# A kernel of attention, SoLU block and mixture of experts: sums and loads of attention moved, tiles turned by halves of their rows

## The reference

```python
# attention: q, k, v are (4, 8, 1152, 64); query pairs are averaged, so 576 queries a head
q_pool = q.reshape(B, H, S // 2, 2, D).mean(axis=3)
scores = scale * np.matmul(q_pool, k.transpose(0, 1, 3, 2))
attn = softmax(scores)                       # with + 1e-09 in the denominator
x = np.matmul(attn, v)                       # then (2304, 512): tokens x features
# SoLU block: w_in (512, 1024), w_out (1024, 512)
h = x @ w_in
solu = h * softmax(h)
x = (layer_norm(solu) * g_ln) @ w_out
# experts: 8 of them, w1 (512, 1024) and w2 (1024, 512) each, a token goes to the best one
out[mask] = gate_w[mask, None] * (np.maximum(x[mask] @ w1[e], 0.0) @ w2[e])
```

## Time and profile before

| | |
|---|---|
| median of 3 runs | 1072.29 us (1070.62 to 1072.95) |
| the profiled execution | 1071.67 us |
| its span, first to last instruction | 1069.6 us |
| mean granted TensorE clock | 0.986 of full |
| busy: TensorE, VectorE, ScalarE, GpSimd | 1012.2, 689.1, 605.1, 409.8 us |

### The profile page before, as it was taken

How to read it: one execution, slowest core, us unless ns; L and a number is a source line. 1 busy time by engine, 2 the same in 40 slices (tenths; PEclk the granted TensorE clock), 3 DMA queues, 4 the chain that set the end, 5 groups by cost and what they waited for, 6 DMA issues and landing times.

```text
span 1069.6 us, 23686 instructions
## 1 busy us (share of the span) xinstructions
PE 1012.2 (95%) x8139; PEld 713.1 (67%) x8139; DVE 689.1 (64%) x1461; ACT 605.1 (57%) x1356; POOL 409.8 (38%) x566
## 2 busy tenths in 40 slices
PE   8699999999999999989999999997999999999996
PEld 5355555555555555545888888876778888888884
DVE  5477777777777777865589999997855513233110
ACT  5477777777777777754654434444556524333231
POOL 3556666565556656673222221152021121111100
PEclk9799999999999999999999999998999999999999
DMA  3432333333332322314300000053665713311100
GB/s 105 110 79 73 83 88 78 88 87 82 84 86 71 81 78 62 108 24 157 91 21 21 30 21 21 21 187 99 245 238 190 269 50 120 119 41 32 40 21 2
DMA packets 97518, 93.66 MB, mean 88 GB/s; under 512 B 49966, under 2 KB 70446, under 8 KB 97264
## 3 DMA queue, kind: packets, MB, share of 16 engines
q1 hardware_dynamic: 93392, 80.79, 25.3%
q0 software_dynamic: 4000, 11.28, 3.2%
HBM read 74.73 MB, written 11.27 MB: 80 GB/s over the span
## 4 chain that ended last, share of the span: by engine, by line
PE 46%; DVE 3%; issue 2%; ACT 1%; POOL 1%; DMA 1%; DVEq 0%; ACTq 0%; POOLq 0%
PE h_ps L771 9%; PE h_ps L773 9%; PE h_ps L772 9%; PE o_ps L771 5%; PE o_ps L773 5%; PE o_ps L772 5%; PE t_ps L1252 2%; PE t_ps L1142 1%; PE h_ps L1219 1%; DVE junk L1348 1%; DMA w_raw_e<-in_moe_w 1%; PE h_ps L1268 1%; DVE w_split L1566 0%; POOL x_lo L1051 0%; ACT w_split L1747 0%
## 5 line engine op out<-in xcount | busy, mean ns | idle before, releaser
L719 ACT ACTIVATE probs<-s_ps,lows 128x576 f32<-128x576 f32 x272 | 199.2, 737 | 88.0 <-DVE lows L603 86.9
L392 POOL TENSOR_SCALAR probs<-probs,raises,recips 128x576 f32<-128x576 f32 x272 | 220.7, 829 | 71.5 <-DVE recips L625 71.5
L603 DVE TENSOR_REDUCE lows<-s_ps 128x1 f32<-128x576 f32 x288 | 204.9, 751 | 62.9 <-PE s_ps L515 55.4
L515 PE MATMUL s_ps<-kt,qt 64*128 64x288 f32 x1024 | 163.2, 435 | 11.1 <-ACT probs L719 9.7
L515 PEld LDWEIGHTS s_ps<-kt,qt 64*128 64x128 f32 x1024 | 88.2, 188 | 113.8 <-ACT probs L719 94.9
L554 PE MATMUL pv_ps<-pt,values 128*64 128x512 f32 x576 | 156.3, 622 | 0.3 <-DVE x_t L647 0.2
L1070 POOL DMA_INDIRECT out<-junk,target_rows x25 | 28.8, 1152 | 261.8 <-ACT junk L1785 261.5
L469 PE MATMUL t_ps<-ident,probs 64*128 64x64 f32 x2178 | 118.9, 226 | 7.4 <-ACT pt L714 5.4
L469 PEld LDWEIGHTS t_ps<-ident,probs 64*128 64x128 f32 x2178 | 104.5, 140 | 22.4 <-DVE pt L632 17.9
L632 DVE COPY pt<-t_ps 128x512 f32<-128x512 f32 x144 | 98.5, 684 | 7.2 <-PE t_ps L469 6.8
L1348 DVE SCALAR_TENSOR_TENSOR junk<-x_rows,emb 128x512 f32<-128x512 f32 x128 | 94.4, 791 | 0.1
(11 more groups left out here) (281 smaller groups left out, 2099.4 us busy)
## 6 DMA issues: line engine op xcount, KB each, us to landing
w_raw_e<-in_moe_w SPq DMA_DIRECT2D x60, 512.0 KB, 5.6
k_raw<-in_k SPq DMA_DIRECT2D x32, 256.0 KB, 2.6
q_raw<-in_q SPq DMA_DIRECT2D x32, 256.0 KB, 3.3
qt<-qx SPq DMA_DIRECT2D x60, 128.0 KB, 2.4
token_rows<-x_rows SPq DMA_DIRECT2D x18, 256.0 KB, 2.0
values<-in_v SPq DMA_DIRECT2D x32, 128.0 KB, 2.7
values<-in_v SPq DMA_DIRECT2D x64, 64.0 KB, 2.6
w_raw<-in_moe_w_in SPq DMA_DIRECT2D x4, 512.0 KB, 5.7
```

Of the source, the lines that this page charges most:

```text
L392: nc.gpsimd.tensor_scalar(where, where, raises[:, par, s, c:c + 1], recips[:, par, s:s + 1], ALU.mult, ALU.mult).then_inc(norm_done if c e ...
L515: last = nc.tensor.matmul(s_ps[c][:, u, 0:part], qt[par][rows(u), s, :], kt[par][rows(u), int(s > full), columns(c)], start=True, stop=True)
L603: nc.vector.tensor_reduce(lows[:, g % 2, s, c:c + 1], s_ps[c][:, :, 0:part], AX.XY, ALU.max, negate=True).then_inc(low_done[c], 1)
L719: nc.scalar.activation(two_halves(probs(g, s)[:])[:, :, columns(c)], s_ps[c][:, :, 0:part], ACT.Exp, bias=lows[:, g % 2, s, c:c + 1], scal ...
```

## The change

In attention the product and the sum of the totals move from GpSimd to VectorE, and the addition of 1e-9 goes into the sum. VectorE now waits for `raises_done` itself, and GpSimd for the reciprocals alone. In VectorE's slot 0 the totals of the last batch of the pair before are written ahead of the loop over batches; no batch has its merge or its totals in slot 0, so the order of what is executed stays. SyncE loads the queries and their tails of pair n first, then the keys of the first head, moves the queries, loads the tail of the keys, the values, and the keys of the second head.

In SoLU and in the experts a tile is turned in 16 transposes of 64 rows by 128 columns instead of 8 of 128 by 128, upper and lower row half in turn. Rows are tokens, so one bank of `t_ps` now holds tokens 0 to 63 of all eight feature blocks, and the other tokens 64 to 127. ScalarE and VectorE copy out by token halves, in strips of 64, into the same `y_hi` and `y_lo`. Both banks are signalled at once. So ScalarE's first copy waits for the whole product of the tile before, the turn for both subtractions of the tile before, and a product for both subtractions of its own tile.

```diff
@@ sync, attention loop
                 if n < pairs:
+                    sp.wait_ge(q_sums, sum_count(n - 1, Q))
+                    load_q(n, 0)
+                    load_q(n, 1)
+                    sp.wait_ge(q_sums, sum_count(n - 1, TAILS))
+                    load_q_tail(n)
                     sp.wait_ge(kq_done, kq_count(n - 1, KA))
                     load_a(n)
                 if at + 1 < pairs:
                     move_queries(at + 1)
+                if n < pairs:
+                    sp.wait_ge(kq_done, kq_count(n - 1, TAILS))
+                    load_k_tail(n)
                 if at < pairs:
                     if at >= 2:
                         sp.wait_ge(pv_done, key_tiles * (at - 1))
                     load_values(at)
                 if n < pairs:
-                    sp.wait_ge(q_sums, sum_count(n - 1, Q))
-                    load_q(n, 0)
-                    load_q(n, 1)
-                    sp.wait_ge(kq_done, kq_count(n - 1, TAILS))
-                    load_k_tail(n)
-                    sp.wait_ge(q_sums, sum_count(n - 1, TAILS))
-                    load_q_tail(n)
                     sp.wait_ge(kq_done, kq_count(n - 1, KB))
                     load_b(n)
@@ gpsimd, normalise
-                steps = 2 * (len(batches) * g + b)
-                pool.wait_ge(raises_done, len(batches) * g + b + 1)
-                pool.sem_inc(passed, 1)
-                nc.gpsimd.tensor_tensor(weighted[:, par, first:end, :], raises[:, par, first:end, :],
-                                        sums[:, par, first:end, :], ALU.mult).then_inc(total_steps, 1)
-                pool.wait_ge(total_steps, steps + 1)
-                pool.sem_inc(passed, 1)
-                nc.gpsimd.tensor_tensor(total[:, par, first:end], weighted[:, par, first:end, 0],
-                                        weighted[:, par, first:end, 1], ALU.add).then_inc(total_steps, 1)
                 pool.wait_ge(recips_done, len(batches) * g + b + 1)
@@ vector, invert_totals
-                dve.wait_ge(total_steps, 2 * (len(batches) * g + b) + 2)
-                nc.vector.tensor_scalar(total[:, par, first:end], total[:, par, first:end], 1e-9, None,
-                                        ALU.add).then_inc(guarded, 1)
-                dve.wait_ge(guarded, len(batches) * g + b + 1)
+                n = len(batches) * g + b + 1
+                dve.wait_ge(raises_done, n)
+                nc.vector.tensor_tensor(weighted[:, par, first:end, :], raises[:, par, first:end, :],
+                                        sums[:, par, first:end, :], ALU.mult).then_inc(weighted_done, 1)
+                dve.wait_ge(weighted_done, n)
+                nc.vector.scalar_tensor_tensor(out=total[:, par, first:end], in0=weighted[:, par, first:end, 0],
+                                               scalar=1e-9, in1=weighted[:, par, first:end, 1], op0=ALU.add,
+                                               op1=ALU.add).then_inc(total_done, 1)
+                dve.wait_ge(total_done, n)
                 nc.vector.reciprocal(recips[:, par, first:end], total[:, par, first:end]).then_inc(recips_done, 1)
@@ build_moe
+        def blocks_of(y, u):
+            return y[:].rearrange("p (b u n) -> p u b n", u=2, n=P // 2)[:, u, :, :]
+
+        def turned_of(u):
+            return t_ps[:, u, :].rearrange("p (b n) -> p b n", n=P // 2)
@@ tensor, down
-                pe.wait_ge(y_lo_done, 2 * m + half + 1)
+                pe.wait_ge(y_lo_done, 2 * m + 2)
@@ tensor, turn and turn_h
+            def turn_by_halves(source, done):
+
+                for f in range(ff_blocks):
+                    for u in range(2):
+                        rows = slice(u * P // 2, (u + 1) * P // 2)
+                        last = nc.tensor.transpose(t_ps[:, u, f * P // 2:(f + 1) * P // 2],
+                                                   source[rows, f * P:(f + 1) * P], ident[rows, rows])
+                last.then_inc(done, 2)
+
             def turn(m):
                 pe.wait_ge(y_ready, m + 1)
-                for half in range(2):
-                    if m >= 1:
-                        pe.wait_ge(y_lo_done, 2 * m - 1 + half)
-                    for i in range(ff_blocks // 2):
-                        f = half * ff_blocks // 2 + i
-                        done = nc.tensor.transpose(t_ps[:, half, i * P:(i + 1) * P],
-                                                   solu[:, m % 2, f * P:(f + 1) * P], ident[:])
-                    done.then_inc(turned, 1)
+                if m >= 1:
+                    pe.wait_ge(y_lo_done, 2 * m)
+                turn_by_halves(solu[:, m % 2, :], turned)
@@ scalar, high_y (low_y, high_h and low_h in the same way)
                 if m >= 1:
-                    act.wait_ge(down_done if half else down_half_done, m)
-                nc.scalar.activation(y_hi[:, half_of(half)], t_ps[:, half, :], ACT.Copy).then_inc(y_hi_done, 1)
+                    act.wait_ge(down_done, m)
+                nc.scalar.activation(blocks_of(y_hi, half), turned_of(half), ACT.Copy).then_inc(y_hi_done, 1)
```

More of the change, by code:

```diff
@@ L154, in build_attention @@
         raises_done = sem("raises_done")
-        total_steps = sem("total_steps")
-        guarded, recips_done = sem("guarded"), sem("recips_done")
+        weighted_done, total_done, recips_done = sem("weighted_done"), sem("total_done"), sem("recips_done")
         half_scaled = sem("half_scaled")
@@ L652, in _ @@
                         lowest(at, s, 1)
+                    if s == 0 and 1 <= at <= pairs:
+                        invert_totals(at - 1, len(batches) - 1)
+                    if at < pairs:
                         for b, (first, end) in enumerate(batches):
@@ L657, in _ @@
                                 invert_totals(at, b)
-                    if s == 0 and 1 <= at <= pairs:
-                        invert_totals(at - 1, len(batches) - 1)
                     if i is not None:
@@ L1245, in turn_h @@
             def turn_h(t):
-                for half in range(halves):
-                    pe.wait_ge(relu_done, halves * t + half + 1)
-                    if t >= 1:
-                        pe.wait_ge(h_lo_done, halves * (t - 1) + half + 1)
-                    for i in range(ff_blocks // 2):
-                        f = half * ff_blocks // 2 + i
-                        done = nc.tensor.transpose(t_ps[:, half, i * P:(i + 1) * P], h[:, f * P:(f + 1) * P], ident[:])
-                    done.then_inc(h_turned, 1)
+                pe.wait_ge(relu_done, halves * (t + 1))
+                if t >= 1:
+                    pe.wait_ge(h_lo_done, halves * t)
+                turn_by_halves(h, h_turned)
             def down_e(t, expert, slot):
@@ L1258, in down_e @@
                     pe.wait_ge(y_copied, t - 1)
+                pe.wait_ge(h_lo_done, halves * (t + 1))
                 for f in range(ff_blocks):
-                    if f % (ff_blocks // 2) == 0:
-                        pe.wait_ge(h_lo_done, halves * t + f // (ff_blocks // 2) + 1)
                     blk, cols = slice(f * P, (f + 1) * P), slice(f % 2 * d_model, (f % 2 + 1) * d_model)
@@ L1377, in low_y @@
                 dve.wait_ge(y_hi_done, 2 * m + half + 1)
-                nc.vector.tensor_tensor(y_lo[:, half_of(half)], t_ps[:, half, :], y_hi[:, half_of(half)].bitcast(F32),
+                nc.vector.tensor_tensor(blocks_of(y_lo, half), turned_of(half), blocks_of(y_hi, half).bitcast(F32),
                                         ALU.subtract).then_inc(y_lo_done, 1)
@@ L1614, in low_h @@
                     dve.wait_ge(h_hi_done, halves * t + n + 1)
-                    nc.vector.tensor_tensor(y_lo[:, half_of(n)], t_ps[:, n, :], y_hi[:, half_of(n)].bitcast(F32),
+                    nc.vector.tensor_tensor(blocks_of(y_lo, n), turned_of(n), blocks_of(y_hi, n).bitcast(F32),
                                             ALU.subtract).then_inc(h_lo_done, 1)
@@ L1777, in high_h @@
                         act.wait_ge(down_e_done, t)
-                    nc.scalar.activation(y_hi[:, half_of(n)], t_ps[:, n, :], ACT.Copy).then_inc(h_hi_done, 1)
+                    nc.scalar.activation(blocks_of(y_hi, n), turned_of(n), ACT.Copy).then_inc(h_hi_done, 1)
             def scale(t):
```

## The result

The changed kernel is slower: a median of 1081.62 us (1080.13 to 1083.39, four runs) beside 1072.45 us of the kernel before on the same chip, a ratio of 1.0089 with an interval of 1.0070 to 1.0109. The forecast was 1051. The profiled execution has a span of 1080.1 us against 1069.6, that is, 10.5 us more.

What follows compares the result with a forecast made beforehand. TensorE was taken to set the pace, losing time in attention to VectorE's waits for GpSimd's totals. The terms -10 - 8 - 3.5 + 0.5 = -21 took 1071.67 to 1051 us; 8-in-10 range 1042 to 1062.

Steps and rivals of the forecast that it cites:

- Start of attention, -10: At the start of attention, queries loaded earlier end the wait for q_sum: -10 us, bounds -8.5 and -11.
- Steady pairs, -8: In attention's steady head pairs, sums on VectorE shorten TensorE's 0.90 us stop: -8 us, bounds 0 and -13.
- last pair, -3.5: In attention's last pair, TensorE's 1.94 us stop and the slow work behind it go: -3.5 us, bounds 0 and -4.
- rival 3: In attention, VectorE's new operations stand behind GpSimd's scalings, so the steady 8 us don't come: 1059 us, chance 0.13.
- Part 3: SoLU and expert turns by row halves: gain 0.17 us a turn, bounds 0 and 0.36, 37 turns, -6.3 us.
- if half turns take over 0.87: Sign that the forecast is wrong: a SoLU or expert half turn, expected at 0.70 us, takes over 0.87.
- parts 3 and 4: SoLU and experts, turning by row halves and handing over whole tiles together: +0.5 us, bounds -6.5 and +7.
- Part 4, tail, +4.7: SoLU's tail: whole-tile hand-over delays the last products and the routing, +4.7 us.
- first SoLU tiles, +1.5: SoLU's first tiles: ScalarE's copy and square come behind the whole product, +1.5 us.
- last expert tile, +0.6: Last expert tile: the product waits for a second subtraction, 0.68 less an overlap of 0.08, +0.6 us.
- Rival 4: SoLU's whole-tile hand-over overruns its 5.6 us cover, so TensorE stops every tile: 1077 us, chance 0.05.

Runs made afterwards that it cites:

- the loads alone: The kernel before with only the changed order of SyncE's loads: 1066.22 us, ratio 0.9939.
- the sums alone: The kernel before with only attention's sums and reciprocals on VectorE, loads in the order of before: 1057.09 us, ratio 0.9850.
- the registers first: The changed kernel with TensorE reading a tile's two registers ahead of the expert turn: 1061.01 us, ratio 0.9900.
- both mends: The changed kernel with expert register reads ahead of the turn and SoLU's last two tiles turned and handed over as before: 1053.02 us, ratio 0.9828.

## Why the prediction was wrong, point by point

- **Start of attention, -10.** The score expected at about 34 came at 35.00, the one expected at 38.6 at 39.96, and 45.98 follows without a low clock. By the rest product the gain is 8.8 us, within the bounds (-8.5 to -11). The split between the parts was not forecast; the runs give 6.0 to the loads alone and 4.0 to the sums alone (63.09), and not quite their sum to both.
- **Steady pairs, -8, and last pair, -3.5.** Right in kind: the 0.90 us stop went, one to two new operations were blocked, and the stop of 0.33 became 0.45 to 0.56 where it occurs (0.68 once, at 449.35), with 0.5 forecast. Since it is absent in five pairs, the gain is 0.9 a pair rather than 0.63: 12.6 us over fourteen intervals, the last pair's first part among them, near the upper bound. From there to the first mark 1.25 us were gained, so the last pair gave less than 3.5 by itself. The sum of attention, -22.6 against -21.5, came out near partly by luck: the start gave 1.2 less than forecast, the steady pairs 4.6 more and the last pair 2.25 less.
- **The blocked operations (rival 3).** The rule of the Trainium skill (SBUF — State Buffer, section "SBUF: two separate sides"), that two such operations lock each other out for a whole instruction, agrees with the 0.62 to 0.77 us above, and with 0.16 where GpSimd stood idle. But it didn't decide: VectorE has room once its wait is gone, as the forecast chose.
- **Part 3, 0.17 a turn: failed.** In SoLU, where nothing else changes, the tile went from 12.07 to 12.04. The marks were unlike. The 0.87 of a full turn runs from its start to where the next product's pace is regular, with the slow step at its end in it; for the half turn I took 0.65 of attention, which has neither edge, and added 0.05. Counted from the last regular product before to the first one behind, less two steps of 0.233, a full turn is 608.72 - 607.38 - 0.466 = 0.87, a half turn 599.39 - 598.08 - 0.466 = 0.84.

Before:

```profile
607.38 0.39 PE L773 MATMUL o_ps<-w_hi,y_lo 128*128 128x512 f32 x1
607.61 1.04 PE L1142 MATMUL t_ps<-ident,solu 128*128 128x128 f32 x8
608.40 0.47 PE L771 MATMUL o_ps<-w_hi,y_hi 128*128 128x512 f32 x1
608.72 0.39 PE L772 MATMUL o_ps<-w_lo,y_hi 128*128 128x512 f32 x1
```

After:

```profile
598.08 0.40 PE L770 MATMUL o_ps<-w_hi,y_lo 128*128 128x512 f32 x1
598.41 0.71 PE L1143 MATMUL t_ps<-ident,solu 64*128 64x64 f32 x16
599.05 0.51 PE L768 MATMUL o_ps<-w_hi,y_hi 128*128 128x512 f32 x1
599.39 0.39 PE L769 MATMUL o_ps<-w_lo,y_hi 128*128 128x512 f32 x1
```

So the turn itself is 0.15 shorter (0.64 against 0.79), and the entry gives 0.10 of it back (0.33 against 0.23). The edge behind it is 0.34 against 0.32. 37 turns are worth 1 us and not 6.3; the measured value lies within the bounds (0 to 0.36), at their foot. The sign of being wrong, "if half turns take over 0.87", did not show: they take 0.84, and that is hardly less.

- **Not in the sum at all: the register reads.** I listed what `turn_h` and `up_e` compute, wait for and hand over, and left out the two reads between them, since the trace of before shows no time for them. That was the missing step: 23 stops of some 0.95, the 22 us of the experts. Part 3 made the turn shorter in time and doubled it in instructions, and I asked only what the turn costs, not what it hid. No rival had it, and the bound of +7 on parts 3 and 4 was too narrow by 26 (1.2, 9.9 and 22.1 us against it).
- **Part 4, tail, +4.7: the waits right, their consequence missed.** They grew by 5.1 us. Another 3.8 are the clock at its lower level after waits of 3.0 and 4.0 us (up to the turning of the last rows it is 24.06 us with the waits bare and 20.29 with them filled, where it was 15.33 before). Some 1.2 more lie in the routing, and the change can't be shown to cause them: from the turning of the last rows to the experts the six kernels with SoLU's code of before take 19.23 to 20.77 us, and the changed one 20.39. The same cost was in the earlier trace rows, at the start and at the last pair, and I counted it there as a gain but not here as a loss.
- **Part 4, first SoLU tiles, +1.5, last expert tile, +0.6.** Both right. Before the product of an early tile TensorE now stands 1.38 us for x_lo (517.56), and from the turn ahead of that product to the next turn it is 13.69 us where it was 12.19. In the last expert tile the product comes 2.96 us after the turn with half turns and 2.34 with full ones.
- **Rival 4.** The sign was its, the mechanism not: no steady SoLU tile waits for y_lo. TensorE is busy all 152 us up to tile 16.

## What to carry to other kernels

When an instruction or a group is replaced by a cheaper one on the bounding engine, list what stands right behind it that costs no time today (here the register reads) and ask whether it was hidden by what goes; if there is such a thing, put it ahead of the group. Measure old and new between the same kinds of mark, from the last regular step before to the first regular one behind. And where an edit adds waits of some microseconds to TensorE, count the clock that they cost as well.

## What the runs showed of the hardware

- Two register reads on TensorE take 1.27 us together (the stops of 0.92 to 1.07 us become 2.19 to 2.30 when they are made twice, and a tile at full clock 14.73 us instead of 13.46). Ahead of a turn or behind 8 full transposes they cost nothing in the steady tiles, behind 16 half ones 0.95 us.
- Stops of 1 us, one in 13.5, left the granted clock at 1.00 (770 to 1050 us). Stops of 2.2 us cost it in some cases and not in others: with one in some 15 us it was 0.93 over 330 us, and thirteen steady tiles of 21 were slow; behind the single one at the end of the experts it was 0.76 for 7 us with the registers first (2.21 us) and with both mends (2.25), and 1.00 in the changed kernel (2.24). With single waits of 3.0 and 4.0 us it was 0.70 from 690 to 695 us and 0.50 from 700 to 705.
- Going from full products to 64-row transposes costs 0.10 us at the entry. Behind either kind of turn the first product step is about 0.1 us long (0.34 and 0.32 against 0.233).
